# Delta-rule solve: n and w as block-diagonal 128x128 tiles instead of two 64x64 tiles

## The chip, the cores and the metric

The kernel runs on one core of one Trainium2 chip. The metric is the device time of one execution in microseconds (us), lower is better. TensorE is PE in the rows (PEld is its weight load), VectorE is DVE, ScalarE is ACT, GpSimd is POOL, SyncE is SP.

## What is computed

Three stages run one behind the other: a delta-rule attention, a gated layer with a product over tokens, and a token and channel mix with sines and cosines. The change is in the first alone:

```python
B, H, S, D = 4, 8, 768, 48
for t in range(S):
    y[:, :, t] = q[:, :, t] @ state
    v_old = state.T @ k_n[:, :, t]
    state = state + beta[t] * outer(k_n[:, :, t], v[:, :, t] - v_old)
```

All is float32 at the interface; k_n is k divided by its norm.

## The kernel before

The attention cuts the 768 tokens into 12 chunks of C = 64. A **unit** u is one chunk of one pair of batches, for all 8 heads: one batch lies on partitions 0 to 63, the other on 64 to 127 (`SIDES = (0, C)`), so there are 24 units. Within a chunk the recurrence is a triangular system: n is the masked product of keys, and its inverse is built by doubling in five levels (`LEVELS = 2, 4, 8, 16, 32`). t and z are the inverse and its transposed partner as far as they are built, w is what one level adds. All four are [128, 8 heads, 64] in float16 (`nh` is n_high, `nl` the remainder of n).

A level l of unit u goes round three engines:
- PE, `level_w` (line 699): n_high times t, a 64x64 product for each of 8 heads and 2 sides, into `t_ps`.
- DVE, `level_w` (line 547): mask it by `lower`, write w.
- PE, `level_tz`: t and z are copied into PSUM by a product with the identity (line 710, 512 columns; for z line 719 at the last level alone), then t gains z times w (line 714) and z gains w times z (line 723), 16 products each.
- ACT `turn` copies the new half of t (line 415, a helper that records all copies of ACT), DVE `level_z` adds z (line 552).

Then `newton` makes one correction step: minus identity times t (line 732) and 32 products of n_rest and n_high with t (line 737), which DVE (line 556) turns into the final t. On PE each product is one weight load and one matmul; products of the two sides use different quarters of the array.

Every engine runs a list written out by hand, one **body** per unit j, with five units in flight: x = j does levels 0 to 2, y = j-1 levels 3 and 4, n = j-2 the newton step, old keys (lines 757, 760) and `solve` (771), v = j-3 the state (782, 787) and outputs (803, 806, 820, 823), f = j+1 the products of keys and queries (`products`, 682, in two halves, masked by DVE at 540) and `first_t` (692), g = j+2 the transposes of keys (`flip`, 669). On PE a body reads: level_w(x,0), products(f,0), level_w(y,3), level_tz(x,0), level_tz(y,3), products(f,1), newton(n), level_w(x,1), level_w(y,4), old_keys(n), level_tz(x,1), level_tz(y,4), z_rests(n) (746), state(v), flip(g,0), old_outputs(v), level_w(x,2), outputs(v), level_tz(x,2), first_t(f), flip(g,1), turn_x(v) (833), solve(n). A unit takes 561 matmuls. Bodies 7 to 12 also split a weight of the next stage on DVE (line 602), and every second body splits x there (607). `norm_setup` runs ahead of the bodies: POOL makes the constants and clears the tiles, DVE and ACT make the key norms.

Of the kernel before, what the change touches and what calls it, by code (L numbers as in the profile page):

```python
# [9 lines left out]
F16 = mybir.dt.float16  # L10
# [100 lines left out]
def norm_setup(nc, whole, k_dram, beta_dram, c, norm_a, norm_b):  # L111
# [3 lines left out]
    with ExitStack() as ctx:  # L115
# [35 lines left out]
        def _(pool):  # L151
# [13 lines left out]
            for a in (c.identf, c.identh):  # L165
                made(nc.gpsimd.memset(a[:], 0.0))
                made(nc.gpsimd.affine_select(out=a[:], in_=a[:], compare_op=ALU.not_equal, fill=1.0, base=0,
                                             pattern=[[-1, P]], channel_multiplier=1))
            for a, one in ((c.ident, 1.0), (c.negident, -1.0)):
                made(nc.gpsimd.memset(a[:], 0.0))  # L170
                select(a[:], ALU.not_equal, one, 0, [[-1, C]], 1)
# [50 lines left out]
def attention(nc, whole, q_dram, k_dram, v_dram, beta_dram, win_dram, xT, norm_a, norm_b, win_raw, win, xs):  # L222

    with ExitStack() as ctx:
# [6 lines left out]
        c.negident = m.sb("neg_ident", [P, C], F16)  # L231
# [4 lines left out]
        c.w = [m.sb(f"w{l}", [P, H, C], F16) for l in range(NL)]  # L236
# [3 lines left out]
        flat += [a[:].rearrange("p h c -> p (h c)") for a in c.w]  # L240
# [5 lines left out]
def delta_rule(nc, ctx, whole, con, q_dram, k_dram, v_dram, win_dram, xT, win_raw, win, xs):  # L246
# [3 lines left out]
    w, knp, kbp = con.w, con.knp, con.kbp  # L250
# [32 lines left out]
    n_high, a_high = m.sem("n_high_made"), m.sem("a_high_made")  # L283
# [129 lines left out]
    def _(act):  # L413
# [70 lines left out]
        for j in bodies:  # L484
# [10 lines left out]
            if live(f):  # L495
                n_highs(f)
            if live(x):
                turn(x, 1)
# [28 lines left out]
    def _(dve):  # L527
# [129 lines left out]
    def _(pe):  # L657
# [37 lines left out]
        def level_w(u, l):  # L695
            pe.wait_ge(t_ready[u % 2], turns_of(u, l - 1))
            for h in range(H):
                for r in SIDES:
                    last = mm(tile(ta[u % 2], r, h), nh[u % NS_][r:r + C, h, :], t[u % TS][r:r + C, h, :],  # L699
                              start=True, stop=True)  # L700
            last.then_inc(w_prod[u % 2], 1)

        def level_tz(u, l):
# [5 lines left out]
            for r in SIDES:  # L709
                mm(ta[u % 2][r:r + C, :], ident[r:r + C, :], t[u % TS][r:r + C].rearrange("p h c -> p (h c)"),  # L710
                   start=True, stop=False, skip_group_check=True)
            for h in range(H):
                for r in SIDES:
                    last = mm(tile(ta[u % 2], r, h), z[u % ZS][r:r + C, h, :], w[l][r:r + C, h, :],  # L714
                              start=False, stop=True, skip_group_check=True)
            last.then_inc(t_prod[u % 2], 1)
            if l == NL - 1:
                for r in SIDES:
                    mm(za[u % 2][r:r + C, :], ident[r:r + C, :], z[u % ZS][r:r + C].rearrange("p h c -> p (h c)"),
                       start=True, stop=False, skip_group_check=True)  # L720
            for h in range(H):
                for r in SIDES:
                    last = mm(tile(za[u % 2], r, h), w[l][r:r + C, h, :], z[u % ZS][r:r + C, h, :],  # L723
                              start=l < NL - 1, stop=True, skip_group_check=True)
            last.then_inc(z_prod[u % 2], 1)

        def newton(u):
# [3 lines left out]
            for r in SIDES:  # L731
                mm(extra[r:r + C, :], negident[r:r + C, :], t[u % TS][r:r + C].rearrange("p h c -> p (h c)"),
                   start=True, stop=False, skip_group_check=True)
            for h in range(H):
                for a in (nl, nh):
                    for r in SIDES:
                        last = mm(tile(extra, r, h), a[u % NS_][r:r + C, h, :], t[u % TS][r:r + C, h, :],
                                  start=False, stop=True, skip_group_check=True)
# [822 lines left out]
```

## Times and profile before

| | us |
|---|---|
| median of 3 runs | 981.45 |
| lowest, highest | 971.77, 982.23 |
| the profiled execution | 978.96 |
| its span in the profile | 977.3 |

Rows of the profile are times on the core's own clock from the span's start. The attention takes about 27 to 470 us of the span, the two dense stages the rest. Rows in order of time merge instructions of one line that follow each other closely: start, time from the first start to the last end, count. A matmul row's time holds its passage through the array, so two rows overlap; what a block costs PE is the distance from its start to the next block's start. "[x <-issue]" is idle time in which PE waited for nothing that the profile shows.

### The profile page before, as it was taken

How to read it: one execution, taken by the hardware profiler on the slowest of the kernel's cores; microseconds unless marked ns; L12 is line 12 of the kernel's file. 1: busy time of each engine (PE TensorE's matmuls, PEld its weight loads, DVE VectorE, ACT ScalarE, POOL GpSimd, SP SyncE). 2: the span in 40 equal slices, each digit the busy share in tenths (PEclk: the TensorE clock that was granted, in tenths of full speed). 3: DMA queues.
4: the chain of work that ended last, by engine and by line, in shares of the span. 5: the costliest groups of instructions: out<-in, count | busy, mean ns of one | idle time of the engine just before them, and what ended most of it. 6: DMA issues, size and time to landing. Idle time of an engine off the chain costs nothing.

```text
span 977.3 us, 35912 instructions
## 1 busy us (share of the span) xinstructions
PE 833.7 (85%) x16080; PEld 779.7 (80%) x16080; DVE 534.4 (55%) x986; ACT 411.7 (42%) x774; POOL 301.0 (31%) x377
## 2 busy tenths in 40 slices
PE   0388777778777887777799999999999999999998
PEld 0277666667666776666599999999999999999998
DVE  4246566666765666654185362552646663744634
ACT  4255546455455564543262332422434433333332
POOL 6787555545545555210050000000001212121120
PEclk9999999999999999998699999999999999999999
DMA  5303111111111111100300000000141010010101
GB/s 198 100 21 99 55 31 58 31 39 50 32 58 31 53 37 32 31 13 11 134 13 1 1 2 0 0 0 1 57 154 33 1 50 1 1 48 0 49 1 49
DMA packets 21471, 38.45 MB, mean 39 GB/s; under 512 B 1744, under 2 KB 15440, under 8 KB 21328
## 3 DMA queue, kind: packets, MB, share of 16 engines
q1 hardware_dynamic: 21328, 36.28, 11.3%
q8 instruction: 122, 2.00, 0.9%
q14 instruction: 21, 0.17, 0.1%
HBM read 31.56 MB, written 4.72 MB: 37 GB/s over the span
## 4 chain that ended last, share of the span: by engine, by line
PE 46%; DVE 2%; issue 1%; ACT 1%; POOL 1%; SPq 0%; POOLq 0%; ACTq 0%
PE dense_ps L922 15%; PE dense_ps L923 15%; PE dense_ps L924 15%; PE dense_ps L1423 1%; PE dense_ps L1422 1%; ACT w_spatial_pair L1126 0%; POOL vn_f L1121 0%; ACT vn_f L1164 0%; DVE vn_f L1340 0%; DVE vn_f L1343 0%; DVE vn_f L1336 0%; POOL vn_f L1119 0%; DVE vn_f L1338 0%; ACT w_out_pair L1126 0%; ACT v_u_pair L1126 0%
## 5 line engine op out<-in xcount | busy, mean ns | idle before, releaser
L1119 POOL TENSOR_TENSOR vn_f<-vn_f 128x384 f32<-128x384 f32 x24 | 24.6, 1023 | 393.7 <-ACT vn_f L1164 393.7
L922 PE MATMUL dense_ps<-w_spatial_pair,vn_pair 128*128 128x384 f32 x336 | 112.2, 334 | 0.0
L923 PE MATMUL dense_ps<-w_spatial_pair,vn_pair 128*128 128x384 f32 x336 | 112.2, 334 | 0.0
L924 PE MATMUL dense_ps<-w_spatial_pair,vn_pair 128*128 128x384 f32 x336 | 112.2, 334 | 0.0
L415 ACT ACTIVATE t<-t_ps 128x256 f16<-128x256 f32 (+1 forms) x144 | 60.1, 418 | 106.1 <-PE t_ps L714 96.8
L547 DVE TENSOR_TENSOR w<-t_ps,lower 128x256 f16<-128x256 f32 x120 | 48.5, 419 | 67.1 <-PE t_ps L699 67.0
L710 PE MATMUL t_ps<-t,ident 64*64 64x512 f16 x240 | 52.6, 405 | 28.4 <-DVE w L547 27.1
L714 PEld LDWEIGHTS t_ps<-w,z 64*64 64x64 f16 x1920 | 57.9, 112 | 18.3 <-issue 8.7
L1349 DVE TENSOR_TENSOR vn_pair<-vn_f,vn_pair 128x384 fp32r<-128x384 f32 x48 | 31.7, 661 | 58.8 <-ACT vn_pair L1126 58.8
L924 PEld LDWEIGHTS dense_ps<-w_spatial_pair,vn_pair 128*128 128x128 f32 x336 | 63.1, 188 | 0.0
L922 PEld LDWEIGHTS dense_ps<-w_spatial_pair,vn_pair 128*128 128x128 f32 x336 | 63.1, 188 | 0.0
L923 PEld LDWEIGHTS dense_ps<-w_spatial_pair,vn_pair 128*128 128x128 f32 x336 | 63.1, 188 | 0.0
L699 PE MATMUL t_ps<-t,n_high 64*64 64x64 f16 x1920 | 58.7, 197 | 4.6 <-issue 4.4
L714 PE MATMUL t_ps<-w,z 64*64 64x64 f16 x1920 | 56.5, 196 | 6.7 <-issue 6.6
L723 PE MATMUL z_ps<-z,w 64*64 64x64 f16 x1920 | 56.5, 196 | 5.2 <-issue 5.1
L552 DVE TENSOR_TENSOR z<-z_ps,z 128x256 f16<-128x256 f32 x96 | 40.3, 419 | 33.2 <-PE z_ps L723 32.9
L1286 DVE BATCH_NORM_STATS2 stats<-v_u_f 128x6 f32<-128x512 f32 x24 | 16.7, 694 | 73.3 <-ACT v_u_f L1185 58.0
L682 PE MATMUL front_ps<-kq,kbT 64*64 64x128 f16 x1152 | 48.7, 231 | 8.8 <-ACT kq L415 7.8
L922 PE MATMUL dense_ps<-w_in_pair,x_pair 128*128 128x512 f32 (+1 forms) x144 | 54.2, 377 | 2.2 <-ACT identr L1126 2.2
L723 PEld LDWEIGHTS z_ps<-z,w 64*64 64x64 f16 x1920 | 47.8, 112 | 7.4 <-issue 5.5
L699 PEld LDWEIGHTS t_ps<-t,n_high 64*64 64x64 f16 x1920 | 47.9, 110 | 6.9 <-issue 5.6
L923 PE MATMUL dense_ps<-w_in_pair,x_pair 128*128 128x512 f32 (+1 forms) x144 | 52.8, 367 | 0.0
(209 smaller groups left out, 2535.1 us busy)
## 6 DMA issues: line engine op xcount, KB each, us to landing
qT_in<-in_q SPq DMA_DIRECT2D x24, 256.0 KB, 3.3
w_in_f<-in_k SPq DMA_DIRECT2D x4, 1152.0 KB, 5.7
k_in<-in_k SPq DMA_DIRECT2D x24, 192.0 KB, 2.7
v_in<-in_v SPq DMA_DIRECT2D x24, 192.0 KB, 2.4
outT<-g_f SPq DMA_DIRECT2D x6, 576.0 KB, 3.1
w_spatial_f<-in_w_spT SPq DMA_DIRECT2D x3, 768.0 KB, 6.1
w_in_f<-in_w_in SPq DMA_DIRECT2D x1, 1536.0 KB, 7.6
w_spatial_f<-in_w_rT SPq DMA_DIRECT2D x3, 384.0 KB, 5.0
```

Source lines behind the costliest of these rows:

```text
L415: return nc.scalar.activation(out, in_, ACT.Copy, scale=scale)
L547: tt(even(w[l], l), odd_even(whole_(ta[u % 2]), l)[:, :, :, 0, :], keep, ALU.mult).then_inc(w_ready[u % 2], 1)
L552: tt(to, odd_even(whole_(za[u % 2]), l)[:, :, :, 1, :], to, ALU.add).then_inc(z_ready[u % 2], 1)
L682: last = mm(front[r:r + C, n * P:n * P + P], kbT[d, b, n, r:r + C], kq[u % KQ][d, o, n, :, r:r + C], start=e == 0, stop=e == 2)
L699: last = mm(tile(ta[u % 2], r, h), nh[u % NS_][r:r + C, h, :], t[u % TS][r:r + C, h, :], start=True, stop=True)
L710: mm(ta[u % 2][r:r + C, :], ident[r:r + C, :], t[u % TS][r:r + C].rearrange("p h c -> p (h c)"), start=True, stop=False, skip_group_check= ...
L714: last = mm(tile(ta[u % 2], r, h), z[u % ZS][r:r + C, h, :], w[l][r:r + C, h, :], start=False, stop=True, skip_group_check=True)
L723: last = mm(tile(za[u % 2], r, h), w[l][r:r + C, h, :], z[u % ZS][r:r + C, h, :], start=l < NL - 1, stop=True, skip_group_check=True)
L922: mm(out, lhs(LO), rhs(HI), start=first, stop=False)
L923: mm(out, lhs(HI), rhs(LO), start=False, stop=False)
L924: return mm(out, lhs(HI), rhs(HI), start=False, stop=last)
L1349: tt(zs[:, LO, r, n], a[:, r], zs[:, HI, r, n].bitcast(F32), ALU.subtract).then_inc(z_rest, 1)
```

## The change

`w` and a new copy of n_high, `nd` (n_diag), become [128, 8, 128]: for each head a 128x128 matrix with the one batch's 64x64 block at the upper left, the other's at the lower right, and zeros elsewhere (cleared once). As the stationary operand such a matrix multiplies both batches' 64 columns in one matmul. This is done for n times t in `level_w` and in `newton`, and for w times z; z times w for t keeps its 64x64 products and reads w's diagonal blocks. The products with the identity also become one matmul over 128 partitions. DVE writes w in two instructions, one for each side, ACT copies n_high into nd in two more.

```diff
         c.negident = m.sb("neg_ident", [P, P], F16)
-        c.w = [m.sb(f"w{l}", [P, H, C], F16) for l in range(NL)]
+        c.w = [m.sb(f"w{l}", [P, H, P], F16) for l in range(NL)]
+        c.nd = [m.sb(f"n_diag{i}", [P, H, P], F16) for i in range(NS_)]
...
-        flat += [a[:].rearrange("p h c -> p (h c)") for a in c.w]
+        flat += [a[:].rearrange("p h c -> p (h c)") for a in (*c.w, *c.nd)]
...
+        def n_diags(u):
+            for r in SIDES:
+                last = copy(nd[u % NS_][r:r + C, :, r:r + C], na[u % 2][r:r + C, :, 0, :])
+            last.then_inc(n_diag, 1)
...
             if live(f):
                 n_highs(f)
+                n_diags(f)
...
-            tt(even(w[l], l), odd_even(whole_(ta[u % 2]), l)[:, :, :, 0, :], keep, ALU.mult).then_inc(w_ready[u % 2], 1)
+            for r in SIDES:
+                to = odd_even(w[l][r:r + C, :, r:r + C], l)[:, :, :, 0, :]
+                last = tt(to, odd_even(whole_(ta[u % 2]), l)[r:r + C, :, :, 0, :], keep[r:r + C], ALU.mult)
+            last.then_inc(w_ready[u % 2], 1)
...
         def level_w(u, l):
             pe.wait_ge(t_ready[u % 2], turns_of(u, l - 1))
+            if l == 0:
+                pe.wait_ge(n_diag, u + 1)
             for h in range(H):
-                for r in SIDES:
-                    last = mm(tile(ta[u % 2], r, h), nh[u % NS_][r:r + C, h, :], t[u % TS][r:r + C, h, :],
-                              start=True, stop=True)
+                last = mm(ta[u % 2][:, h * C:h * C + C], nd[u % NS_][:, h, :], t[u % TS][:, h, :], start=True, stop=True)
...
-            for r in SIDES:
-                mm(ta[u % 2][r:r + C, :], ident[r:r + C, :], t[u % TS][r:r + C].rearrange("p h c -> p (h c)"),
-                   start=True, stop=False, skip_group_check=True)
+            mm(ta[u % 2][:], con.identh[:], t[u % TS][:].rearrange("p h c -> p (h c)"),
+               start=True, stop=False, skip_group_check=True)
...
-                    last = mm(tile(ta[u % 2], r, h), z[u % ZS][r:r + C, h, :], w[l][r:r + C, h, :],
+                    last = mm(tile(ta[u % 2], r, h), z[u % ZS][r:r + C, h, :], w[l][r:r + C, h, r:r + C],
...
             for h in range(H):
-                for r in SIDES:
-                    last = mm(tile(za[u % 2], r, h), w[l][r:r + C, h, :], z[u % ZS][r:r + C, h, :],
-                              start=l < NL - 1, stop=True, skip_group_check=True)
+                last = mm(za[u % 2][:, h * C:h * C + C], w[l][:, h, :], z[u % ZS][:, h, :],
+                          start=l < NL - 1, stop=True, skip_group_check=True)
...
             for h in range(H):
-                for a in (nl, nh):
-                    for r in SIDES:
-                        last = mm(tile(extra, r, h), a[u % NS_][r:r + C, h, :], t[u % TS][r:r + C, h, :],
-                                  start=False, stop=True, skip_group_check=True)
+                mm(extra[:, h * C:h * C + C], nd[u % NS_][:, h, :], t[u % TS][:, h, :],
+                   start=False, stop=False, skip_group_check=True)
+            for h in range(H):
+                for r in SIDES:
+                    last = mm(tile(extra, r, h), nl[u % NS_][r:r + C, h, :], t[u % TS][r:r + C, h, :],
+                              start=False, stop=True, skip_group_check=True)
```

On PE, the end of a body (`outputs`, then level_tz(x,2), first_t, flip(g,1)) reads before:

```order
L710 MATMUL t_ps<-t,ident 64x512 x2
L714 MATMUL t_ps<-w,z 64x64 x16
L723 MATMUL z_ps<-z,w 64x64 x16
L692 MATMUL t_ps<-ident,z 64x64 x16
L669 MATMUL front_ps<-identh,kn_pair 128x128 x8
```

and in the changed kernel (line 718 is the old 710, 722 the old 714, 729 the old 723, 701 the old 692, 678 the old 669):

```order
L718 MATMUL t_ps<-t,identh 128x512
L722 MATMUL t_ps<-w,z 64x64 x16
L729 MATMUL z_ps<-z,w 128x64 x8
L701 MATMUL t_ps<-ident,z 64x64 x16
L678 MATMUL front_ps<-identh,kn_pair 128x128 x8
```

Two blocks of five now use the whole array where one did, and the array's division changes four times in this piece (64 to 128 at 718, to 64 at 722, to 128 at 729, to 64 at 701, and once more at 678 as before).

The middle of a body on PE, from level_tz(y,3) over newton to level_w(y,4), reads in the changed kernel (691 is `products`, 737, 740 and 744 are newton, 709 is level_w):

```order
L718 MATMUL t_ps<-t,identh 128x512
L722 MATMUL t_ps<-w,z 64x64 x16
L729 MATMUL z_ps<-z,w 128x64 x8
L691 MATMUL front_ps<-kq,kbT 64x128 x24
L737 MATMUL extra_ps<-t,neg_ident 128x512
L740 MATMUL extra_ps<-t,n_diag 128x64 x8
L744 MATMUL extra_ps<-t,n_rest 64x64 x16
L709 MATMUL t_ps<-t,n_diag 128x64 x16
```

where before all of it was 64-row tiles, with 32 products of n_rest and n_high mixed, and 32 of level_w.

On DVE, the same place (the mask of the second half, newton, level_w(x,1), level_w(y,4), the first of r_full) reads in the changed kernel (before, each w line was one instruction over 128 partitions):

```order
L546 TENSOR_TENSOR na<-front_ps,mask 128x512
L565 TENSOR_TENSOR t<-ident,extra_ps 128x512
L555 TENSOR_TENSOR w<-t_ps,lower 64x8x8x4 x2
L555 TENSOR_TENSOR w<-t_ps,lower 64x8x32 x2
L573 SCALAR_TENSOR_TENSOR rf<-v_in,side_ps 128x384
```

Nothing moves to another place on DVE; each w takes two instructions of 64 partitions with as many elements in each partition as before.

## Rows read from the trace of the kernel before

**Rows 1.** The page: busy tenths of PE in 40 equal slices of the span.
```profile
PE   0388777778777887777799999999999999999998
```

**Rows 2.** Stretch totals: length, busy us (x instructions) by engine, granted clock, DMA share, GB/s.
```profile
110.00:425.00 315.00, 246.59 (x10107) 217.44 (x10108) 201.09 (x397) 167.94 (x339) 157.81 (x188) 0.97 0.14 40
```

**Rows 3.** PEld waits, 110 to 425 us: waiter, releaser, total us, times, longest.
```profile
PEld t_ps L710 <- DVE w L547: 22.3, 28, 3.0
...
PEld side_ps L771 <- issue: 7.2, 24, 1.0
...
PEld front_ps L682 <- issue: 0.4, 1, 0.4
```

**Rows 4.** PE in order of time around one pause: start, us, instruction, [idle before].
```profile
304.78 0.35 PE L746 MATMUL extra_ps<-z,t 64*64 64x64 f16 x10
306.55 0.24 PE L746 MATMUL extra_ps<-z,t 64*64 64x64 f16 x3 [1.42 <-issue]
```

**Rows 5.** The view of Rows 2 for stretches from one pause to the next.
```profile
255.29:259.56 4.27, 2.82 (x127) 2.39 (x126) 3.24 (x6) 2.58 (x5) 0.92 (x1) 1.00 0.31 107
...
333.63:337.19 3.56, 2.81 (x127) 2.59 (x127) 2.34 (x5) 1.01 (x2) 1.36 (x3) 1.00 0.02 5
337.19:340.99 3.79, 2.63 (x126) 2.50 (x126) 2.13 (x5) 1.97 (x5) 2.23 (x4) 1.00 0.23 63
```

**Rows 6.** DMA queues, 60 to 450 us: packets, MB, share.
```profile
q8 instruction: 98, 1.61, 1.8%
```

**Rows 7.** PE in order of time, 240 to 242 us.
```profile
240.12 0.40 PE L710 MATMUL t_ps<-t,ident 64*64 64x512 f16 x2
240.36 0.41 PE L714 MATMUL t_ps<-w,z 64*64 64x64 f16 x16
240.61 0.42 PE L723 MATMUL z_ps<-z,w 64*64 64x64 f16 x16
240.87 0.42 PE L692 MATMUL t_ps<-ident,z 64*64 64x64 f16 x16
241.22 0.62 PE L669 MATMUL front_ps<-identh,kn_pair 128*128 128x128 f16 x8
241.67 0.50 PE L833 MATMUL extra_ps<-identf,yf 128*128 128x128 f32 x3
242.10 0.21 PE L771 MATMUL side_ps<-rl_pair,z_rest 64*64 64x48 f16 x2
```

**Rows 8.** PEld by form, 240 to 420 us: shape and count, busy us, mean ns, idle.
```profile
L714 PEld LDWEIGHTS t_ps<-w,z 64*64 64x64 f16 x832 | 25.8, 110 | 6.0 <-issue 2.0
...
L669 PEld LDWEIGHTS front_ps<-identh,kn_pair 128*128 128x128 f16 x88 | 4.9, 98 | 0.5
```

**Rows 9.** PE in order of time, one body.
```profile
383.91 0.75 PE L682 MATMUL front_ps<-kq,kbT 64*64 64x128 f16 x20 [0.59 <-ACT kq L415]
...
386.49 0.40 PE L710 MATMUL t_ps<-t,ident 64*64 64x512 f16 x2 [0.75 <-DVE w L547]
...
387.69 0.40 PE L732 MATMUL extra_ps<-t,neg_ident 64*64 64x512 f16 x1
...
390.03 0.40 PE L710 MATMUL t_ps<-t,ident 64*64 64x512 f16 x2 [0.16 <-DVE w L547]
```

**Rows 10.** DVE in order of time, the same body.
```profile
388.95 0.69 DVE L556 TENSOR_TENSOR t<-ident,extra_ps 128x512 f16<-128x512 f16 x1 [0.16 <-PE extra_ps L737]
389.55 0.75 DVE L547 TENSOR_TENSOR w<-t_ps,lower 128x256 f16<-128x256 f32 x2
```

**Rows 11.** ACT in order of time, the same body.
```profile
388.83 0.63 ACT L415 ACTIVATE n_high<-na 128x512 f16<-128x512 f32 x1 [1.26 <-DVE na L540]
390.72 0.38 ACT L415 ACTIVATE t<-t_ps 128x256 f16<-128x256 f32 x1 [1.27 <-PE t_ps L714]
```

**Rows 12.** POOL in order of time, start of the program.
```profile
17.40 1.32 POOL L185 MEMSET w<- 128x256 f32 x5
29.48 0.83 POOL L392 TENSOR_TENSOR kn<-k_in,rnorm 128x384 f32<-128x384 f32 x1 [10.76 <-DMA k_in<-in_k]
```

More of the change, by code:

```diff
@@ L163, in select @@
                                                  channel_multiplier=up))
-            for a in (c.identf, c.identh):
+            for a, one in ((c.identf, 1.0), (c.identh, 1.0), (c.negident, -1.0)):
                 made(nc.gpsimd.memset(a[:], 0.0))
-                made(nc.gpsimd.affine_select(out=a[:], in_=a[:], compare_op=ALU.not_equal, fill=1.0, base=0,
+                made(nc.gpsimd.affine_select(out=a[:], in_=a[:], compare_op=ALU.not_equal, fill=one, base=0,
                                              pattern=[[-1, P]], channel_multiplier=1))
-            for a, one in ((c.ident, 1.0), (c.negident, -1.0)):
-                made(nc.gpsimd.memset(a[:], 0.0))
-                select(a[:], ALU.not_equal, one, 0, [[-1, C]], 1)
+            made(nc.gpsimd.memset(c.ident[:], 0.0))
+            select(c.ident[:], ALU.not_equal, 1.0, 0, [[-1, C]], 1)
             made(nc.gpsimd.memset(c.band[:], 1.0))
@@ L230, in attention @@
         c.identh = m.sb("identh", [P, P], F16)
-        c.negident = m.sb("neg_ident", [P, C], F16)
+        c.negident = m.sb("neg_ident", [P, P], F16)
         c.identf = m.sb("identf", [P, P])
@@ L282, in delta_rule @@
     na_prod, na_masked = m.sem("na_prod"), m.sem("na_masked")
-    n_high, a_high = m.sem("n_high_made"), m.sem("a_high_made")
+    n_high, n_diag, a_high = m.sem("n_high_made"), m.sem("n_diag_made"), m.sem("a_high_made")
     w_prod, w_ready = m.sems("w_prod"), m.sems("w_ready")
@@ L717, in level_tz @@
             if l == NL - 1:
[L718 to L720 removed]
+                mm(za[u % 2][:], con.identh[:], z[u % ZS][:].rearrange("p h c -> p (h c)"),
+                   start=True, stop=False, skip_group_check=True)
             for h in range(H):
[L722 to L724 removed]
+                last = mm(za[u % 2][:, h * C:h * C + C], w[l][:, h, :], z[u % ZS][:, h, :],
+                          start=l < NL - 1, stop=True, skip_group_check=True)
             last.then_inc(z_prod[u % 2], 1)
@@ L730, in newton @@
             need(pe, x_out, u - 1)
-            for r in SIDES:
-                mm(extra[r:r + C, :], negident[r:r + C, :], t[u % TS][r:r + C].rearrange("p h c -> p (h c)"),
-                   start=True, stop=False, skip_group_check=True)
+            mm(extra[:], negident[:], t[u % TS][:].rearrange("p h c -> p (h c)"),
+               start=True, stop=False, skip_group_check=True)
             for h in range(H):
-                for a in (nl, nh):
-                    for r in SIDES:
-                        last = mm(tile(extra, r, h), a[u % NS_][r:r + C, h, :], t[u % TS][r:r + C, h, :],
-                                  start=False, stop=True, skip_group_check=True)
+                mm(extra[:, h * C:h * C + C], nd[u % NS_][:, h, :], t[u % TS][:, h, :],
[4 more added lines that the diff above has]
+                              start=False, stop=True, skip_group_check=True)
             last.then_inc(new_prod, 1)
```

2 lines of the change are left out of this document (1 added, 1 removed).

## The prediction

> **What bounds the kernel now.** The slices of the page come first: PE is busy 7 to 8 tenths in the attention (slices 3 to 19) and 9 or more behind it [rows 1]. Nothing of the change lies behind the attention, so I leave the second half alone. The stretch totals give the length of a body: from 110 to 425 us PE ran 10107 matmuls [rows 2], at 561 a unit 18.0 bodies, so 17.5 us a body.
>
> The waits of PE's weight loads then say what fills the gaps [rows 3]. In 315 us, 22.3 us go to w from DVE, and there are sixteen groups "issue", in which PE waited for nothing that the profile shows; of them the first and the last stand in the rows, and all sixteen sum to 42.5 us. About 3 us of that is a regular 0.17 us before `solve`, so 39.6 us, or **2.2 us a body**, are pauses in the middle of blocks. In time order such a pause looks like this: ten of the 16 products of line 746 run, then 1.42 us of nothing, then the same line goes on [rows 4]. The reader should see that no semaphore can stop a block there.
>
> What ends the pauses is seen by counting from one to the next: 126 or 127 matmuls with 126 or 127 weight loads each time, in stretches of 3.56 to 4.27 us [rows 5]. With the few separate waits of PE that makes 256 instructions. The DMA view has a queue of instructions: 98 packets and 1.61 MB in 390 us [rows 6], so 16.4 KB every 3.98 us, which is 256 instructions of 64 bytes. So PE's program comes in blocks of 256, a block takes 3.6 to 4.3 us to come (I use 3.9), and where PE runs through one faster it pauses. A body has 1122 matmuls and loads, 1137 instructions with waits, 4.44 blocks: 4.44 times 3.9 is 17.3 us, nearly the whole body. Two limits lie close together: the supply at 17.3, and the work with its waits for DVE and ACT at 17.5 - 2.2 = 15.3 us.
>
> The Trainium skill says otherwise ("Runtime: NRT & Kernel Launch", section Instruction fetch mechanics): blocks of 16 KiB are fetched ahead and crossing a boundary is mostly hidden. The block size agrees with the trace, the hiding does not. By that rule the pauses would have another cause and would stay; this is a rival below.
>
> **What the change takes away.** 95 matmuls and 95 loads of 1122, so a body has 932 + 15 = 947 instructions, 3.70 blocks, 14.4 us of supply. The work will be longer than that, so the pauses go: up to -2.2 us a body. How much work a body has afterwards decides.
>
> **What it does to PE's own work.** In order of time a block of 16 64x64 products costs 0.25 us: from line 723 at 240.61 to line 692 at 240.87 [rows 7], 31 ns for a pair on the two sides, since the pair runs side by side. One 128x128 matmul of 64 columns takes its place. The nearest row is line 669, eight of 128x128 with 128 columns in 0.45 us, 56 ns each [rows 7]. Streaming 64 columns in place of 128 gives half of that, about 29 ns, if the weight load is hidden, and 56 ns if it is not. That is from below as well, since 56 ns for 128 columns is 0.44 ns a column and 28 ns for 64. I take 29 to 30 ns, since the load of 128x128 is shown no longer than that of 64x64 (98 against 110 ns) [rows 8]. So 8 cost 0.24 us where 16 cost 0.25: **the halved count gives PE nearly nothing**. The identity's 512 columns cost one stream before and after.
>
> The page "TensorE: Matmul & The Clock Gate", section Weight-path perf modes, of the Trainium skill has a fast load for full 128-column weights that are not float32, and "TensorEngine Tiling (Array Packing)", section Performance Considerations, says column tiling turns it off; the order of the two load times agrees. By it the sum stays as it is.
>
> What costs is the change of the array's division. Line 692 (64x64) to 669 (128x128) took 0.35 us where the 16 products need 0.25 [rows 7]. That is 0.10 in rounded rows; I take 0.095 us for each change, either way (the step back from 833 to 771 in the same rows can't be split). "TensorEngine Tiling (Array Packing)", section Tiling Modes, states that a change of mode drains the engine; the row agrees. Before, a body had 4 changes, around the two flips. By the order afterwards it has 28. Of the 24 new ones:
> - 10 are hidden. Two around level_w(x,0), since PE then waits 0.59 us for kq from ACT [rows 9]; three in level_w(y,3) and level_tz(x,0), since PE then waits 0.75 us for w [rows 9]; three around level_w(x,1) and old_keys and two around outputs, where PE ends while DVE is still making w. Without that cover they would cost 1.0 us.
> - 14 are on the path: 3 in level_tz(y,3) and before products, 2 in newton, 5 in level_tz(x,1), level_tz(y,4) and before z_rests, 1 before level_w(x,2), 3 in level_tz(x,2) and before first_t. 14 x 0.095 = 1.33 us; the smaller blocks give back about 0.11.
>
> **DVE.** Each w becomes two instructions, with as many elements in a partition. The trace has no DVE instruction on 64 partitions; between nothing and a full second one, I take the full one: two w back to back take 0.75 us, one 0.41, so 0.34 more [rows 10]. Three of five are waited for: w of level 3 (tz waits 0.75 us [rows 9]); w of level 1, where newton's end, DVE's 0.69 us and w release line 710 at 390.03 with a wait of 0.16 [rows 9, 10]; w of level 2 likewise (line 710 waited for w 28 times in 18 bodies [rows 3]). 3 x 0.34 = 1.02 us. Level 0 has the cover of kq, level 4 comes behind 0.7 us of level_tz(x,1).
>
> **ACT and POOL.** Two more copies of at most 0.63 us each stand behind n_high, in front of the copy of t at 390.72: n_high starts at 388.83, the t copy came 1.27 us after the last work ended [rows 11]; 388.83 + 0.6 + 1.2 ends at 390.6, before it. Nothing, and if the cover fails at most 0.3 us, since t of level 1 itself comes later by the DVE term. nd is used a body later. POOL clears some 3 us more at the start (5 tiles of 256 take 1.32 us [rows 12]) but then idles 10.76 us: nothing.
>
> **The sum.** Work of a body: 15.3 + 1.33 - 0.11 + 1.02 = 17.5 us. Some blocks of 256 will still come late: over the densest piece (level_w(x,1) to state) they take about 4.0 us against 3.6 to 4.3 of supply; I add 0.1. So 17.6 against 17.5: the pauses are filled with switches and DVE halves. 18 bodies x 0.1 = +2 us. The first and last bodies have few pauses and the same new work, some +3 us in all. 978.96 (the profiled execution, 1.7 outside its span) + 5 = **984 us**. The median shown is 2.5 higher than that execution and the runs spread over 10 us, so this is no change that could be seen.
>
> **Rivals.**
> - *Cover is better than I count* (0.25). Changes of division or DVE's second half cost less on the path. Without the changes' 1.33: 16.3 us, -1.2 x 18 = 957 us. If the DVE term also goes: 15.2, near the supply, 940. For it: every unhidden switch I have is next to a transposing block. Against: 0.35 to 0.25 is plain.
> - *The 128x128 load is not hidden* (0.17). 56 in place of 29 ns, 0.21 us a block, six blocks on the path (z in four level_tz, n in newton, level_w(x,2)): +1.3 us a body, 1007 us. The step from 29 to 56 decides. Against: the load times.
> - *The pauses stay* (0.08). They follow something else than the count of instructions. Then 2.2 us a body on top: +40 us and the ends, 1022 us. Against: 253 matmuls and loads between pauses each time. The skill's rule named above would have it so.
> - *A lower clock* (0.05). The granted clock was 0.97 and PE busy 246.59 us, 13.7 a body [rows 2]; at 0.90 that grows by up to 1.1 us: 984 + 19 = 1003 us. Against: fewer pauses speak for no less clock.
>
> **How the numbers follow.** My forecast holds 0.45 with its own range 972 to 996. The range for 8 in 10 reaches to the first rival's 957 and just over the second's 1007: 957 to 1010. About 1% (10 us) is what can be told from no change here. Faster by more than that, under 972: 0.27, from the first rival and the low edge of mine; slower, over 991: 0.34, from the others and my upper edge; between: 0.39.
>
> **What would show it.** Right: few "issue" pauses, the instruction queue at more than 4.2 us a packet, a body near 17.5 us, the block of line 729 near 0.24 us, 0.09 to 0.1 us between blocks of unlike division, w in two rows 0.34 apart, waits for w about as long as before. Wrong: 729 near 0.45 us; pauses of 2 us a body still there; a body of 16 us.

## The result, and the profile after

| | before | after |
|---|---|---|
| median of 4 runs, us | 981.84 | 1014.55 |
| the profiled execution | 978.96 | 1013.53 |
| its span | 977.3 | 1011.5 |

The ratio is 1.037 (95%: 1.028 to 1.046): **slower by 33 us**. The forecast was 984 with a range to 1010, so the time lies outside the range, on the slow side. Every count below is against the two profiled executions (34.2 us apart in their spans). One run each of two kernels below, at 1345 and at 1094 us with a mean granted clock of 0.57 and 0.75, stood in a slower state and is left out of their times.

The page of the kernel after, its shares and the slices; the slices of PE answer to [rows 1]:

```profile
PE 885.9 (88%) x13800; PEld 791.7 (78%) x13800; DVE 596.5 (59%) x1106; ACT 438.6 (43%) x822; POOL 302.7 (30%) x380
...
PE   0378888878888888888789999999999999999998
...
PEclk9999999887799999997679999999999999999999
```

PE runs 13,800 matmuls, 2280 fewer than before, and is busier in the attention than in [rows 1], and the clock it was granted dips in slices 8 to 11, where [rows 2] had 0.97 over the whole stretch. The stretch totals of the kernel after, the same stretch as [rows 2], then the dense stages:

```profile
110.00:425.00 315.00, 266.91 (x7745) 211.01 (x7743) 230.99 (x451) 173.91 (x348) 155.78 (x186) 0.92 0.13 38
...
510.00:1011.00 501.00, 494.21 (x2811) 482.56 (x2811) 258.87 (x462) 177.39 (x320) 63.23 (x55) 0.99 0.08 29
```

and the dense stages of the kernel before:

```profile
475.00:977.00 502.00, 494.28 (x2811) 482.65 (x2811) 258.57 (x462) 177.38 (x321) 63.26 (x55) 0.99 0.08 29
```

7745 matmuls at 466 a unit are 16.6 bodies in 315 us: **18.95 us a body, where it was 17.5**. Behind the attention nothing moved: 2811 matmuls kept PE busy for 494.21 and 494.28 us. So all 34 us were lost in the attention.

The waits of PE's weight loads in the kernel after, 110 to 425 us (waiter, releaser, total us, times, longest), answer to [rows 3]:

```profile
PEld t_ps L718 <- DVE w L555: 35.2, 44, 3.1
PEld t_ps L722 <- issue: 21.3, 84, 0.4
PEld side_ps L810 <- DVE state L598: 13.9, 16, 0.9
...
PEld side_ps L778 <- issue: 2.7, 16, 0.2
PEld extra_ps L740 <- issue: 1.9, 7, 0.3
PEld extra_ps L737 <- issue: 1.2, 7, 0.2
```

The pauses in the middle of blocks are gone. What is still called "issue" at line 722 is 0.25 us 84 times, always behind the identity's 512 columns: it is the length of that stream, now one matmul on all rows, and no stall. In the place of the pauses stands a longer wait for w: 35.2 us in 16.6 bodies where 22.3 stood in 18.0.

The DMA view of the kernel after, 60 to 450 us, answers to [rows 6]:

```profile
q8 instruction: 75, 1.23, 1.2%
```

390 us for 75 blocks is 5.2 us a block, where it was 3.98: PE no longer runs against the supply.

PE of the kernel after in order of time, one body (start, us, instruction, [idle before]), answers to [rows 7] and [rows 9]:

```profile
307.00 0.39 PE L718 MATMUL t_ps<-t,identh 128*128 128x512 f16 x1 [0.89 <-DVE w L555]
307.32 0.44 PE L722 MATMUL t_ps<-w,z 64*64 64x64 f16 x16
307.69 0.41 PE L729 MATMUL z_ps<-z,w 128*128 128x64 f16 x8
308.03 0.86 PE L691 MATMUL front_ps<-kq,kbT 64*64 64x128 f16 x24
308.82 0.39 PE L737 MATMUL extra_ps<-t,neg_ident 128*128 128x512 f16 x1
309.05 0.40 PE L740 MATMUL extra_ps<-t,n_diag 128*128 128x64 f16 x8
309.37 0.44 PE L744 MATMUL extra_ps<-t,n_rest 64*64 64x64 f16 x16
309.75 0.64 PE L709 MATMUL t_ps<-t,n_diag 128*128 128x64 f16 x16
...
311.37 0.39 PE L718 MATMUL t_ps<-t,identh 128*128 128x512 f16 x1 [0.40 <-DVE w L555]
```

From start to start a block of 8 at 128x128 takes 0.32 or 0.34 us with the change of division behind it (line 740 to 744, 729 to 691); without it, it would be 0.23, since single matmuls of line 709 next to each other start 29 ns apart. A block of 16 at 64x64 takes 0.37 or 0.38 with its change (722 to 729, 744 to 709), where [rows 7] had 0.25. Among the single starts of the trace, the first matmul behind a change comes 125 ns after the last one ahead of it when the division goes from 64x64 to 128x128 and 123 ns on the way back, where like ones are 28 or 29 ns apart: 0.095 us each way, as the sum had it.

The same weight loads by form in the kernel after, 240 to 420 us (shape and count, busy us, mean ns, idle), answer to [rows 8]:

```profile
L722 PEld LDWEIGHTS t_ps<-w,z 64*64 64x64 f16 x800 | 17.1, 112 | 12.7 <-issue 12.7
L729 PEld LDWEIGHTS z_ps<-z,w 128*128 128x128 f16 x393 | 15.6, 100 | 2.8
```

The load of 128x128 is hidden behind the matmul before it: 100 ns each, at one matmul every 31 ns. DVE of the kernel after in order of time, the same body, answers to [rows 10]:

```profile
309.86 0.69 DVE L565 TENSOR_TENSOR t<-ident,extra_ps 128x512 f16<-128x512 f16 x1 [0.23 <-PE extra_ps L744]
310.46 1.74 DVE L555 TENSOR_TENSOR w<-t_ps,lower 64x256 f16<-64x256 f32 x4
312.23 0.56 DVE L573 SCALAR_TENSOR_TENSOR rf<-v_in,side_ps 128x384 f32<-128x384 f32 x1
```

Two w of four instructions occupy DVE 1.74 us, 0.44 each, and the next work starts 1.77 us after the first. In the kernel before, the two w of [rows 10] start at 389.55, and the work behind them is this:

```profile
390.22 0.54 DVE L564 SCALAR_TENSOR_TENSOR rf<-v_in,side_ps 128x384 f32<-128x384 f32 x1
```

That is 0.67 us for two w, so one w keeps the next work of DVE waiting **0.55 us longer** (0.88 for 0.33). A single w is finished some 0.43 us later (0.85 for 0.42). The sum had 0.34.

### The profile page after: what moved, and what is told of

Same layout as the page of the kernel before. It is cut to its first block and busy times, and to the rows that moved or that the text cites. A ratio compares the mean times of both kernels' runs of the same rounds, so it can differ in the third digit from the quotient of the medians.

```text
span 1011.5 us, 31546 instructions
## 1 busy us (share of the span) xinstructions
PE 885.9 (88%) x13800; PEld 791.7 (78%) x13800; DVE 596.5 (59%) x1106; ACT 438.6 (43%) x822; POOL 302.7 (30%) x380
## 5 line engine op out<-in xcount | busy, mean ns | idle before, releaser
L555 DVE TENSOR_TENSOR w<-t_ps,lower 64x256 f16<-64x256 f32 x240 | 100.8, 420 | 57.0 <-PE t_ps L709 54.6
L718 PE MATMUL t_ps<-t,identh 128*128 128x512 f16 x120 | 49.9, 416 | 45.3 <-DVE w L555 45.3
L722 PEld LDWEIGHTS t_ps<-w,z 64*64 64x64 f16 x1920 | 41.7, 113 | 31.1 <-issue 31.1
L561 DVE TENSOR_TENSOR z<-z_ps,z 128x256 f16<-128x256 f32 x96 | 40.7, 424 | 30.9 <-PE z_ps L729 29.8
L929 PE MATMUL dense_ps<-w_in_pair,x_pair 128*128 128x512 f32 (+1 forms) x144 | 54.2, 377 | 2.2 <-ACT identr L1133 2.2
L718 PEld LDWEIGHTS t_ps<-t,identh 128*128 128x128 f16 x120 | 11.8, 99 | 53.7 <-DVE w L555 52.9
L931 PE MATMUL dense_ps<-w_in_pair,x_pair 128*128 128x512 f32 (+1 forms) x144 | 52.8, 367 | 0.0
L930 PE MATMUL dense_ps<-w_in_pair,x_pair 128*128 128x512 f32 (+1 forms) x144 | 52.8, 366 | 0.0
L691 PEld LDWEIGHTS front_ps<-kq,kbT 64*64 64x64 f16 x1152 | 39.3, 120 | 16.1 <-ACT kq L415 13.6
L729 PE MATMUL z_ps<-z,w 128*128 128x64 f16 x960 | 51.4, 199 | 0.0
```

Of the source, the lines that this page charges most:

```text
L555: last = tt(to, odd_even(whole_(ta[u % 2]), l)[r:r + C, :, :, 0, :], keep[r:r + C], ALU.mult)
L561: tt(to, odd_even(whole_(za[u % 2]), l)[:, :, :, 1, :], to, ALU.add).then_inc(z_ready[u % 2], 1)
L691: last = mm(front[r:r + C, n * P:n * P + P], kbT[d, b, n, r:r + C], kq[u % KQ][d, o, n, :, r:r + C], start=e == 0, stop=e == 2)
L718: mm(ta[u % 2][:], con.identh[:], t[u % TS][:].rearrange("p h c -> p (h c)"), start=True, stop=False, skip_group_check=True)
L729: last = mm(za[u % 2][:, h * C:h * C + C], w[l][:, h, :], z[u % ZS][:, h, :], start=l < NL - 1, stop=True, skip_group_check=True)
L929: mm(out, lhs(LO), rhs(HI), start=first, stop=False)
```

## The experiments

The theory after the result was that DVE's second instruction and what it makes late (waits of PE, then a lower clock) cost the time, while the pauses did go and the division changes cost what they should. The rivals: the division changes cost more than counted; the 128x128 products do; the pauses were no matter of the number of instructions.

### DVE's split alone

Before, with w written in two instructions of 64 partitions; PE's work is untouched.

```diff
-            tt(even(w[l], l), odd_even(whole_(ta[u % 2]), l)[:, :, :, 0, :], keep, ALU.mult).then_inc(w_ready[u % 2], 1)
+            for r in SIDES:
+                to = odd_even(w[l][r:r + C, :, :], l)[:, :, :, 0, :]
+                last = tt(to, odd_even(whole_(ta[u % 2]), l)[r:r + C, :, :, 0, :], keep[r:r + C], ALU.mult)
+            last.then_inc(w_ready[u % 2], 1)
```

> The kernel before, with DVE's masking of w alone split into two instructions of 64 partitions, PE untouched. Theory 1 (PE's program comes in blocks of 256 instructions every 3.9 us, and the changed kernel lost because its own work grew past that): the split adds 0.45 to 0.55 us at three waits of a body, but most of it fills pauses, so 985 to 997 us, with fewer pauses than before. Rival (DVE's second half alone is the loss): 1010 us or more. Rival (the split costs nothing): 981 us.

It took 1000.26 us against 982.87, ratio 1.017 (1.011 to 1.022), 3 us above the 985 to 997 that were expected. The waits of PE's weight loads in this kernel, 110 to 425 us:

```profile
PEld t_ps L713 <- DVE w L549: 47.7, 50, 3.4
PEld side_ps L806 <- DVE state L592: 15.8, 16, 1.1
...
PEld side_ps L774 <- issue: 3.6, 21, 0.2
```

The wait for w doubled, from the 22.3 us of [rows 3] to 47.7, and of the 42.5 us of "issue" before, 15.6 are left in all groups: while PE waits for w, its program catches up. At 17.4 bodies in the stretch (9757 matmuls) these are 1.50 us more and 1.46 us less a body, so the pauses pay for the new wait. A body is still 0.6 us longer: 0.26 are in the waits for state and kq, and the clock was 0.95 for 0.97. In the kernel after, no pause is left to pay, so the same split should cost more there; the fourth experiment measures it.

### Fewer instructions alone

Before, with 88 matmuls a unit fewer and no change of division: a matmul of 128 columns serves two heads with the matrix of the first, so the second head does not get its own product.

```diff
         def level_w(u, l):
...
-            for h in range(H):
+            for h in range(0, H, 2):
                 for r in SIDES:
-                    last = mm(tile(ta[u % 2], r, h), nh[u % NS_][r:r + C, h, :], t[u % TS][r:r + C, h, :],
-                              start=True, stop=True)
+                    last = mm(ta[u % 2][r:r + C, h * C:h * C + 2 * C], nh[u % NS_][r:r + C, h, :],
+                              t[u % TS][r:r + C, h:h + 2, :].rearrange("p h c -> p (h c)"), start=True, stop=True)
```

The same is done in z's product of `level_tz` and for n_high in `newton`.

> The kernel before, with 88 fewer matmuls a unit and no change of the array's division: n times t, w times z and newton's n_high times t take two heads' columns (128) for one head's stationary tile, so half the heads get the wrong matrix; the streamed columns stay the same. Theory 1: a body goes from 4.44 blocks of 256 instructions to 3.75, the work stays at 15.2 us, so the 2.2 us of pauses mostly go: 935 to 950 us. Rival (the pauses follow something else than the count of instructions): 975 to 982 us.

It took 945.43 us, ratio 0.962 (0.955 to 0.969): **37 us come back**. The stretch totals of this kernel:

```profile
110.00:425.00 315.00, 255.61 (x9281) 224.71 (x9279) 220.75 (x431) 176.87 (x366) 157.75 (x187) 0.96 0.14 41
```

9281 matmuls at 473 a unit are 19.6 bodies of 16.05 us, 1.4 less than before. Of the 39.6 us of pauses about 11 are left in this stretch, though the columns streamed are the same, DVE and ACT do the same work, and PE waits longer for w (30.9 us for 22.3). So the pauses follow the count of instructions. A little of the gain is array time: z's block of 8 matmuls with 128 columns takes 0.23 us where 16 with 64 took 0.25, which is at most 0.26 of the 1.4 us in ten such blocks a body. The result speaks against the Trainium skill's "Runtime: NRT & Kernel Launch", section Instruction fetch mechanics, by which the crossing of a block is mostly hidden; here it is hidden only while PE needs longer for 256 instructions than the 3.6 to 4.3 us from one pause to the next in [rows 5].

### The same, with the identity's products over 128 partitions

The kernel above, and t's identity product as one 128x128 matmul, as the change has it: 5 matmuls fewer, 10 more changes of division.

```diff
-            for r in SIDES:
-                mm(ta[u % 2][r:r + C, :], ident[r:r + C, :], t[u % TS][r:r + C].rearrange("p h c -> p (h c)"),
-                   start=True, stop=False, skip_group_check=True)
+            mm(ta[u % 2][:], con.identh[:], t[u % TS][:].rearrange("p h c -> p (h c)"),
+               start=True, stop=False, skip_group_check=True)
```

> b_two_heads (946.3 us; half the heads get the wrong matrix) with the five copies of t by the identity as one 128x128 matmul each: 5 matmuls fewer and 10 changes of the array's division more a body, nothing else. 5 of the 10 stand where PE waits for w anyway. If only those on the path count: 5 x 0.093 x 22 = +10, less some 3 for 10 instructions fewer: 951 to 958 us. If each of the ten counts: 963 to 967 us. If changes of division cost nothing and d_one_write's distance to b_two_heads (33 us) is something else: 943 to 947 us.

It took 947.77 us (ratio to before 0.968, 0.964 to 0.972), 2.3 more than the kernel above. That is less than the 951 to 958 that the on-path count wanted, and within 1 us of the time expected if changes of division cost nothing. The waits for "issue" of this kernel, all there are in 110 to 425 us:

```profile
PEld t_ps L713 <- issue: 22.6, 98, 0.4
PEld side_ps L775 <- issue: 3.8, 21, 0.4
PEld side_ps L824 <- issue: 0.7, 2, 0.4
PEld side_ps L791 <- issue: 0.2, 1, 0.2
```

The kernel above still had about 11 us of pauses in that stretch (3.4 at line 714, 1.9 at 792, 1.5 at 699 and so on); here they are gone and the identity's stream has come. A body is 16.06 us where it was 16.05, so the likely reading is that the changes of division filled the pauses that were left, and that they cost where no pause is left to fill. The next kernel and the passages further below show such places.

### The whole change with w written at once

After, with w written by one instruction of 128 partitions. w is then not block-diagonal, so the two batches mix in w times z; every instruction of PE and ACT is that of the change.

```diff
-            for r in SIDES:
-                to = odd_even(w[l][r:r + C, :, r:r + C], l)[:, :, :, 0, :]
-                last = tt(to, odd_even(whole_(ta[u % 2]), l)[r:r + C, :, :, 0, :], keep[r:r + C], ALU.mult)
-            last.then_inc(w_ready[u % 2], 1)
+            to = odd_even(w[l][:, :, 0:C], l)[:, :, :, 0, :]
+            tt(to, odd_even(whole_(ta[u % 2]), l)[:, :, :, 0, :], keep, ALU.mult).then_inc(w_ready[u % 2], 1)
```

> The changed kernel, with w written by DVE in one instruction of 128 partitions into the left half of each head's tile, so that w is not block-diagonal and the values are not those of the reference; PE, ACT and the order are those of the change. Theory 1: 0.45 to 0.55 us less at three waits of a body and less DVE work in bodies 7 to 12, where the clock fell: 1014 - 24 x 1.5 = 978, with the clock back 965 to 982 us. Rival (the changes of division are the loss, DVE's second half is covered): 1005 to 1015 us.

It took 979.69 us, ratio 0.996 (0.993 to 0.998). Two things follow. From the kernel after to this one are 34.9 us, which is **what DVE's second instruction costs in the changed kernel**. And the rest of the change, fewer instructions against 24 more changes of division (with ACT's copies of n_high), comes out even: -37 from the one, +34 from the other. The 34 are 1.4 us for each of 24 bodies, where the sum had 1.33 - 0.11 on the path, but this nearness is in part luck, since they do not lie evenly. Against the kernel of the second experiment 7 us lie ahead of the first `solve` and 14.5 in bodies 7 to 12, and each of bodies 13 to 20 is only 0.5 us longer (16.2 for 15.7). So the price of a change is not read from this difference, but from the single starts above and the passages below. PE of this kernel in body 12:

```profile
254.74 0.39 PE L716 MATMUL t_ps<-t,identh 128*128 128x512 f16 x1 [2.56 <-DVE w L554]
```

With w in one instruction too, PE waits 2.56 us for it there.

### DVE's two splits moved out of the way

In bodies 7 to 12 DVE splits a weight and in every second body x, just ahead of the mask and of level 3's w. Both kernels below have these two put at the end of DVE's body, once with the change and once without.

```diff
-            if live(v - 1) and pair_of(v - 1) == 0:
-                x0_rests(v - 1)
-            if 0 <= j - WIN_BODY - 1 < 2 * KX:
-                win_rests(j - WIN_BODY - 1)
...
             if live(x):
                 level_z(x, 2)
+            if live(v - 1) and pair_of(v - 1) == 0:
+                x0_rests(v - 1)
+            if 0 <= j - WIN_BODY - 1 < 2 * KX:
+                win_rests(j - WIN_BODY - 1)
```

With the change:

> The changed kernel with two pieces of DVE work (the split of the next stage's weight in bodies 7 to 12, the split of x in every second body) moved from in front of w of level 3 to the end of the body, where DVE waits 2 us for PE. If these bodies lost because the longer DVE chain left PE idle and its clock fell (a body took 20.9 us there against 17.6 elsewhere), they come back to 17.5: 1014 - 6 x 3.3 - 12 x 0.2 = 985 to 995 us. Rival (their length comes from PE's own work at the lower clock, which falls for another reason): 1008 us or more.

Without it:

> The same move in the kernel before. There the supply of instructions (4.44 blocks of 3.9 us) bounds a body at 17.3 us whatever DVE does: 972 to 981 us, much less than the move gives the changed kernel. Rival (DVE's chain was the bound of the kernel before too): 955 to 965 us.

With the change it took 991.32 us (ratio to before 1.007, 1.004 to 1.010), 23 us less than the kernel after; without it 977.94 (0.995, 0.992 to 0.999), 4.5 less than before. So the pile-up in front of level 3's w costs five times as much in the changed kernel. Whether w's second instruction does that, or the rest of the change, the starts of `solve` in each trace tell (mean length of a body from one `solve` to the next, us):

| kernel | first `solve` at | bodies 7 to 12 | bodies 13 to 20 |
|---|---|---|---|
| before | 84.5 | 17.9 | 17.2 |
| before, w in two instructions | 90.0 | 19.3 | 17.5 |
| after, w in one | 91.4 | 19.4 | 16.2 |
| after | 89.4 | 21.1 | 17.7 |
| after, the two splits moved | 92.0 | 17.5 | 17.2 |

It is both: each alone makes bodies 7 to 12 1.4 or 1.5 us longer, and together they make them 3.2 longer. The likely reason for the part of PE is that in the kernel before its program caught up during these waits and later pauses were shorter, while the changed kernel has no pause to shorten. Where the time goes is in the traces. DVE of the kernel after in order of time, one of the six bodies:

```profile
223.39 1.03 DVE L616 TENSOR_TENSOR x_pair<-xT,x_pair 128x192 fp32r<-128x192 f32 x1
224.34 1.40 DVE L611 TENSOR_TENSOR w_in_pair<-w_in_f,w_in_pair 128x512 fp32r<-128x512 f32 x1
225.66 0.68 DVE L546 TENSOR_TENSOR na<-front_ps,mask 128x512 f32<-128x512 f32 x1
226.26 0.84 DVE L555 TENSOR_TENSOR w<-t_ps,lower 64x256 f16<-64x256 f32 x2
```

PE of the same body, and in the next fence the stretch totals around it (clock in the third column from the end):

```profile
227.16 0.61 PE L718 MATMUL t_ps<-t,identh 128*128 128x512 f16 x1 [3.00 <-DVE w L555]
227.70 0.63 PE L722 MATMUL t_ps<-w,z 64*64 64x64 f16 x16
228.27 0.61 PE L729 MATMUL z_ps<-z,w 128*128 128x64 f16 x8
228.81 1.49 PE L691 MATMUL front_ps<-kq,kbT 64*64 64x128 f16 x24
```

```profile
219.00:226.00 7.00, 4.65 (x143) 3.79 (x140) 4.45 (x8) 4.18 (x9) 5.78 (x7) 1.00 0.01 2
226.00:233.00 7.00, 5.84 (x98) 4.56 (x100) 3.75 (x9) 2.16 (x4) 1.22 (x3) 0.53 0.01 2
233.00:240.00 7.00, 6.06 (x212) 4.78 (x206) 6.32 (x13) 4.12 (x9) 2.51 (x3) 0.98 0.32 100
```

PE waits 3.00 us for w, and then runs at a mean clock of 0.53 (almost all of it at 1.2 GHz in place of 2.4): 98 matmuls in 7 us where 212 follow. The block of line 722 takes 0.57 us to the next in place of 0.37. Such a stretch, 3 to 9 us of half clock, follows the wait for level 3's w in each of the six bodies, after a wait of 3.00 us in three of them and 1.45 in the others. One more, of 6.9 us, follows a wait of only 0.89 us at 376.7 us; its body takes 20.0 us in place of 17.1, and waits as long in other bodies have none. In the kernel before, the same place had waits of 1.70, 2.86 and 2.79 us in the three bodies with both splits, and fewer and shorter falls of the clock; two stretches of the kernel before:

```profile
210.00:216.00 6.00, 3.85 (x115) 3.61 (x116) 3.80 (x7) 1.01 (x2) 1.60 (x3) 0.73 0.01 3
246.00:252.00 6.00, 3.30 (x158) 3.03 (x158) 5.06 (x10) 1.02 (x2) 2.21 (x4) 1.00 0.01 3
```

The 2.86 us are in the first, the 2.79 in the second. So a long wait alone doesn't tell whether the clock falls, and what else decides stays open. With the splits moved, PE's longest wait for w is 1.2 us and the clock stays up. The stretch totals of that kernel, the change with both splits moved:

```profile
110.00:425.00 315.00, 272.68 (x8417) 216.41 (x8413) 245.78 (x489) 188.17 (x378) 158.86 (x193) 0.99 0.13 39
```

8417 matmuls are 18.06 bodies of **17.44 us: the 17.5 of the sum**. The kernel before, with both splits moved:

```profile
110.00:425.00 315.00, 250.39 (x10151) 221.50 (x10150) 195.53 (x397) 169.07 (x341) 155.56 (x188) 0.96 0.14 40
```

10151 matmuls are 18.09 bodies of 17.41 us. In the middle of the attention the two are equal; the 13.4 us between their medians lie at its ends. The first `solve` starts at 92.0 us with the change and at 82.8 without, the last one at 480.7 and 465.5. The waits there say why. PE early in the kernel before, and then at the same place in the kernel after:

```profile
67.61 0.40 PE L710 MATMUL t_ps<-t,ident 64*64 64x512 f16 x2 [0.61 <-DVE w L547]
70.89 0.40 PE L710 MATMUL t_ps<-t,ident 64*64 64x512 f16 x2 [0.52 <-DVE w L547]
```

```profile
69.15 0.39 PE L718 MATMUL t_ps<-t,identh 128*128 128x512 f16 x1 [0.98 <-DVE w L555]
73.05 0.39 PE L718 MATMUL t_ps<-t,identh 128*128 128x512 f16 x1 [0.98 <-DVE w L555]
```

While few units are in flight PE waits for w at every level, so every second half stands on the path, 0.4 us each, and not three in a body.

### The second instruction, split by columns instead

The kernel before, with w in two instructions of all 128 partitions and half the heads each. Is it the second instruction that costs, or the half of the partitions?

```diff
-            tt(even(w[l], l), odd_even(whole_(ta[u % 2]), l)[:, :, :, 0, :], keep, ALU.mult).then_inc(w_ready[u % 2], 1)
+            for h in (0, HP):
+                to = odd_even(w[l][:, h:h + HP, :], l)[:, :, :, 0, :]
+                last = tt(to, odd_even(whole_(ta[u % 2]), l)[:, h:h + HP, :, 0, :], keep[:, h:h + HP], ALU.mult)
+            last.then_inc(w_ready[u % 2], 1)
```

> The kernel before with DVE's masking of w split by heads instead of sides: two instructions of 128 partitions and half the columns. a_dve_split (two of 64 partitions and all columns) took 1000.3 us, a start-to-start distance of 0.44 us and 0.89 us for a w. If the second instruction costs by columns, the pair's distance is 0.20 to 0.25 us and the time 982 to 988 us. If it costs by being an instruction whatever its size: 0.4 us and 995 to 1002 us.

It took 987.14 us (ratio 1.004, 1.001 to 1.007), 4 to 5 us of loss where the split by partitions had 17. DVE of this kernel in order of time, and behind it DVE of the kernel with the split by partitions:

```profile
303.99 0.49 DVE L549 TENSOR_TENSOR w<-t_ps,lower 128x128 f16<-128x128 f32 x2 [2.66 <-PE t_ps L702]
```

```profile
308.44 0.85 DVE L549 TENSOR_TENSOR w<-t_ps,lower 64x256 f16<-64x256 f32 x2
309.32 0.56 DVE L597 TENSOR_TENSOR state_pair<-state,state_pair 128x384 f16<-128x384 f32 x1
```

A pair by columns takes 0.49 us, a pair by partitions 0.85 and 0.88 to the next start, one whole instruction 0.42 [rows 10 has two in 0.75]. The duration goes by the elements in a partition, and half the partitions save nothing.

### A smaller change

What the runs so far say together: take away instructions, leave w in one piece. nd is made by ACT off the path, so its use needs nothing of DVE. First n_diag in `level_w` alone:

```diff
             for h in range(H):
-                for r in SIDES:
-                    last = mm(tile(ta[u % 2], r, h), nh[u % NS_][r:r + C, h, :], t[u % TS][r:r + C, h, :],
-                              start=True, stop=True)
+                last = mm(ta[u % 2][:, h * C:h * C + C], nd[u % NS_][:, h, :], t[u % TS][:, h, :], start=True, stop=True)
```

> Of the change only n_diag and the products of level_w with it: 40 fewer matmuls a unit, w and newton as before, DVE as before. 8 new changes of the array's division, 7 of them where PE waits for DVE or ACT anyway. Theory 1: 4.13 blocks a body are 16.1 us of supply against 15.3 us of work: 950 to 968 us. Rival (every change of division costs 0.095 us wherever it stands, and pauses stay): 8 x 0.095 x 22 = +17, 998 us.

It took 965.87 us, ratio 0.982 (0.977 to 0.987). With DVE's two splits moved as well:

> n_diag in level_w alone (as c_level_w_only, 965.9 us) with the same move of DVE work. Supply 4.13 blocks, 16.1 us a body; work 15.2 us less 0.5 in bodies 7 to 12: 953 to 963 us. Rival (move and count don't add, since the supply already bounds): 964 to 968 us.

958.56 us, 0.973 (0.969 to 0.978). And with n_diag in `newton` too, put behind the 16 products of n_rest, next to `level_w`, so that `newton` has one change of division in place of two:

```diff
             for h in range(H):
-                for a in (nl, nh):
-                    for r in SIDES:
-                        last = mm(tile(extra, r, h), a[u % NS_][r:r + C, h, :], t[u % TS][r:r + C, h, :],
-                                  start=False, stop=True, skip_group_check=True)
+                for r in SIDES:
+                    mm(tile(extra, r, h), nl[u % NS_][r:r + C, h, :], t[u % TS][r:r + C, h, :],
+                       start=False, stop=False, skip_group_check=True)
+            for h in range(H):
+                last = mm(extra[:, h * C:h * C + C], nd[u % NS_][:, h, :], t[u % TS][:, h, :],
+                          start=False, stop=True, skip_group_check=True)
```

> As h_level_w_moved, and newton's n_high times t with n_diag, put last in newton so that level_w(x,1) follows in the same division of the array: 8 matmuls fewer still (3.99 + 0.08 blocks), no further change of division, one of the existing ones now on the path (0.095 us). 0.24 us less supply and 0.1 more work a body: 2 to 5 us below h_level_w_moved where the supply still bounds, the same where it doesn't.

**950.88 us, ratio 0.965 (0.961 to 0.969), faster than both kernels**, by 32 us than before and by 64 than after. It is 7.7 us below the kernel ahead of it, where 2 to 5 were expected; the runs of the two touch each other (946 to 953 and 953 to 960). The stretch totals of this kernel:

```profile
110.00:425.00 315.00, 272.02 (x9968) 233.17 (x9966) 210.16 (x427) 199.77 (x402) 158.22 (x190) 0.98 0.14 41
```

At 513 matmuls a unit that is 19.4 bodies of 16.2 us.

## Why the prediction was wrong

The forecast was a near balance: pauses of 2.2 us a body filled by 2.2 us of new work, alike in all bodies. The whole has these parts (medians of the runs, us):

| step | time | of it |
|---|---|---|
| before | 982.9 | |
| fewer instructions, no new division changes | 945.4 | -37 |
| all of PE's and ACT's part of the change | 979.7 | +34 |
| DVE's two instructions as well | 1014.6 | +35 |

- **The pauses**: right. They follow the number of instructions and went with it. No "issue" in the middle of a block is left, and the queue is at 5.2 us a block.
- **The block of 8**: right. 29 ns a matmul, the load hidden; the rival of 56 ns is out. (What the prediction draws on for column tiling stands under "Restrictions" on that page of the Trainium skill, "TensorEngine Tiling (Array Packing)"; the load times, 98 ns at 128x128 and 110 at 64x64, agree in their order.)
- **The division changes**: right in price and in the count of those on the path. In the table below (passages between the same points in bodies without a pause, from the starts of single matmuls in both traces) the three that hold changes alone grew by 1.33 us where the sum had 1.25.
- **DVE's second instruction: the step that failed.** It was taken as 0.34 us, half of a back-to-back pair of the old shape, in three places, 1.02 us a body. The passages with a w grew by 0.44, 0.51 and 0.55, together 1.50 for 1.12 with the one change among them, and the whole kernel lost 35 us by it, 1.45 a body. The price alone is 0.38 us a body, 7 us over 18 bodies, which would have left the time inside the range.
- **One body for all: the step that took the time out of the range.** The sum multiplied one body by 18 and took PE's wait for level 3's w from a body where it is 0.75 us, though [rows 3] has a wait of 3.0. In bodies 7 to 12 that w stands behind the splits of weight and x. With the change PE stops for it 1.45 or 3.00 us and then runs at half its clock, and probably no pause is left that this could shorten: 3.2 us more a body there, where the sum had 0.1.
- **The ends**: mis-sized. The first and last bodies were put at 3 us together; they cost 11, since every level waits for its w there.
- **ACT and POOL** at nothing: no row speaks against it. PE's waits for ACT are 8.3 us for kq in the stretch, 5.9 before.

| passage of a body | before | after | more | in the sum |
|---|---|---|---|---|
| newton's end to level_tz (x,1), w of level 1 | 1.31 | 1.75 | 0.44 | 0.34 |
| to the end of state (5 changes) | 2.41 | 2.91 | 0.50 | 0.48 |
| old_outputs' start to level_tz(x,2), w of level 2 and a change | 1.43 | 1.94 | 0.51 | 0.44 |
| to turn_x (3 changes) | 1.55 | 1.86 | 0.31 | 0.29 |
| products(f,0) to level_tz(y,3), w of level 3 | 2.07 | 2.62 | 0.55 | 0.34 |
| on to newton's end (3 + 2 changes) | 2.10 | 2.62 | 0.52 | 0.48 |

All of them together grew by 2.8 us where the sum had 2.37 (less the 0.11 that the smaller blocks give back). An undisturbed body of the kernel after is 17.1 to 17.7 us, as forecast; the six bodies 7 to 12 took 21.1 on average, where before they took 17.9. So of the 34 us, 19 are in these six bodies, 4 in the other twelve of the middle 18, 5 in the bodies ahead of them and 6 behind. Taken from another point of the body, the six have 17 and the twelve 6. The forecast had about 1, 1 and, for the two ends, 3.

Which rival held? Not one alone. "A lower clock" had 0.05 and gave 1003: the clock was 0.92 in this stretch, and the argument against it, that fewer pauses speak for no less clock, did not hold. It looked at pauses and not at the waits that take their place. The clock and the stall can't be told apart fully: moving the splits takes both away, 23 us against 4.5 in the kernel before, so 18 to 19 us belong to the stall with the clock together. An estimate for the clock alone: the mean fell from 0.97 to 0.92, so 0.05 / 0.5 x 315 = 31 us more stand at half, and newton takes PE 1.36 us there and 0.80 otherwise; 31 x (1 - 0.80 / 1.36) is some 13 us at most, as waits don't stretch.

The range failed at its upper end because no term stood for bodies unlike the one that was read, and the DVE term had no range besides. It was taken "between nothing and a full second one" of the old shape, so the top of the bound was the price itself; a 64-partition form was in no row, and it could cost more than the row next to it.

## What to carry to other kernels

Fewer TensorE instructions were worth 37 us where PE's program came too slowly in blocks of 256, as long as they were not paid for with changes of division on the path or on another engine. A layout that spares one engine half of its instructions may make another write in two halves: count what stands in front of that write in every body, the odd ones first, since there the new piece lands on a stall. And a stall that cost little while the engine had other pauses to shorten can cost its full length once they are gone: here the same DVE work, moved out of the way, gave 4.5 us before the change and 23 after it. A price is bounded from above only by a row of a dearer form, not by the nearest one.

## What the hardware showed

- DVE takes as long on 64 partitions as on 128 with the same elements in each: 420 ns for 64x256 and 419 for 128x256. But back to back the whole ones start 0.34 us apart [rows 10] and the halves 0.44, so a following half doesn't overlap the one before. Why is open.
- A change of the array's division costs PE 0.095 us each way (125 and 123 ns from start to start, 28 or 29 between like ones). Ten more of them in a body left its length as it was, 16.06 for 16.05 us, while the pauses in which PE stood still for its program went from 11 us to 1 in the stretch.
- After a wait of 1.45 or 3.00 us for w PE ran 3 to 9 us at half its clock, in six of six bodies of the kernel after. In the kernel before, a wait of 2.79 us went without it. What decides is open.
